# Up product turned round: x stationary, split w_in moving in steps of 512 columns, g transposed behind Mish, and w_out split by TensorE

## The reference

```python
scores = 0.125 * q @ k.T                       # per batch and head, 576 x 576
kth    = 32nd largest score of each row
attn   = softmax(where(scores >= kth, scores, -1e9))
x      = (attn @ v) as 2304 tokens x 512
h      = x @ w_in                              # w_in 512 x 2048
g      = h * tanh(softplus(h))                 # Mish
y      = g @ w_out                             # w_out 2048 x 512
```

## Time and profile before

| | us |
|---|---|
| median of 3 runs | 761.02 (760.97 to 761.91) |
| the profiled execution | 761.13 |
| its span (first to last instruction) | 759.3 |
| busy PE / PEld / DVE / ACT / POOL | 720.5 / 625.3 / 700.5 / 570.3 / 494.3 |

### The profile page before, as it was taken

The page is one execution under the profiler, slowest core; times in us unless marked ns, Lnnn a source line. Parts: engine busy times, 40 slices in busy tenths (PEclk is TensorE's granted clock), DMA queues, the critical chain, the costliest instruction groups (busy, mean ns, idle before and its releaser), DMA issues.

```text
span 759.3 us, 16003 instructions
## 1 busy us (share of the span) xinstructions
PE 720.5 (95%) x6056; PEld 625.3 (82%) x6056; DVE 700.5 (92%) x1512; ACT 570.3 (75%) x942; POOL 494.3 (65%) x590
## 2 busy tenths in 40 slices
PE   4258999999999999999999999999999999999998
PEld 2147888888989898979898989898888888888987
DVE  5999999999999999999999999999999999999600
ACT  3576978787879787878787777878796969687831
POOL 1877858576766666666667585848585858585813
PEclk9998999999999999999999999999999999999999
DMA  7560000031230000111110000001122000000000
GB/s 273 179 214 14 8 22 8 22 104 57 66 102 9 12 20 8 40 33 38 47 52 8 23 8 22 9 22 43 57 78 91 6 22 8 22 2 15 1 15 15
DMA packets 22684, 34.06 MB, mean 45 GB/s; under 512 B 2384, under 2 KB 11600, under 8 KB 22096
## 3 DMA queue, kind: packets, MB, share of 16 engines
q1 hardware_dynamic: 22608, 33.04, 13.3%
HBM read 28.31 MB, written 4.72 MB: 43 GB/s over the span
## 4 chain that ended last, share of the span: by engine, by line
PE 92%; DVE 6%; DMA 0%; issue 0%; ACT 0%; POOL 0%; SPq 0%
PE ps_u L397 35%; PE ps_y L412 27%; PE ps_o L379 10%; PE ps_s L351 9%; PE ps_s L332 9%; DVE left L601 3%; DVE top L607 2%; PE ps_o L372 1%; PE ps_s L328 1%; DVE top L592 1%; DMA q_sb<-q_in 0%; POOL p_sb L674 0%; ACT x_sb L459 0%; ACT xT L499 0%; ACT y_sb L528 0%
## 5 line engine op out<-in xcount | busy, mean ns | idle before, releaser
L607 DVE MAX8 top<-left 128x8 f32<-128x576 f32 x432 | 304.8, 747 | 0.0
L397 PEld LDWEIGHTS ps_u<-xT,win 128*128 128x128 f32 x2304 | 262.5, 192 | 13.8 <-issue 11.1
L397 PE MATMUL ps_u<-xT,win 128*128 128x128 f32 x2304 | 271.8, 277 | 0.7 <-ACT xT L499 0.7
L601 DVE MATCH_REPLACE8 left<-top,left 128x576 f32<-128x576 f32 x288 | 211.8, 743 | 0.0
L659 POOL TENSOR_TENSOR p_sb<-x_sb,p_sb 128x576 f32<-128x576 f32 x144 | 202.4, 1422 | 8.5 <-ACT p_sb L469 8.4
L489 ACT ACTIVATE pT<-ps_s 128x512 f32<-128x512 f32 (+1 forms) x144 | 85.6, 646 | 71.1 <-PE ps_s L351 71.1
L478 ACT ACTIVATE p_sb<-p_sb,neg_max 128x576 f32<-128x576 f32 x144 | 110.6, 769 | 27.7 <-POOL p_sb L659 27.2
L674 POOL TENSOR_SCALAR p_sb<-p_sb,recip 128x576 f32<-128x576 f32 x144 | 106.2, 747 | 35.6 <-DVE recip L582 35.6
L412 PE MATMUL ps_y<-w_hi,g_hi 128*128 128x512 f32 x288 | 117.9, 409 | 0.0
L469 ACT ACTIVATE p_sb<-x_sb,limit 128x576 f32<-128x576 f32 x144 | 105.5, 772 | 12.6 <-POOL limit L649 12.5
L412 PE MATMUL ps_y<-w_hi,g_lo 128*128 128x512 f32 x288 | 112.5, 391 | 0.0
(11 more groups left out here) (30 smaller groups left out, 603.5 us busy)
## 6 DMA issues: line engine op xcount, KB each, us to landing
v_sb<-v_in SPq DMA_DIRECT2D x32, 320.0 KB, 3.5
k_sb<-k_in SPq DMA_DIRECT2D x16, 288.0 KB, 3.3
q_sb<-q_in SPq DMA_DIRECT2D x68, 64.0 KB, 1.8
g_raw<-w_out SPq DMA_DIRECT2D x8, 512.0 KB, 4.4
win<-w_in SPq DMA_DIRECT2D x4, 1024.0 KB, 8.9
y_out<-y_sb SPq DMA_DIRECT2D x16, 256.0 KB, 2.0
y_out<-y_sb SPq DMA_DIRECT2D x4, 128.0 KB, 2.3
q_sb<-q_in SPq DMA_DIRECT2D x1, 256.0 KB, 3.4
```

The source lines that it names most:

```text
L397: mm = pe.matmul(ps_u[:, n % 2, i, :], win[:, k, P * f:P * f + P], xT[:, k, :], start=(k == 0), stop=(k == KC - 1), skip_group_check=True)
L601: dve.match_replace(out=left[:, t, :], in_to_replace=best[:, t, EIGHT * r:EIGHT * r + EIGHT], in_values=x[t] if r == 0 else left[:, t, :], ...
L607: dve.max(best[:, t, EIGHT * r + EIGHT:EIGHT * r + 2 * EIGHT], left[:, t, :]).then_inc(found, 1)
```

## The change

- Up product: `xT` is split into `xT_hi` and `xT_lo` (fp32r, POOL) and is now the weights; w_in is split into `win_hi` and `win_lo`, and moves in steps of 512 columns. One `up(m, j)` is 12 fp32r matmuls of 512 columns and yields token-major sums.
- Mish reads 1024 columns from PSUM and writes `g_tok`; `turn(m, j)` on PE transposes four tiles each (16 a block) back into `ps_u`; `copy_g(m, j)` on ACT copies 512 columns into `raw`, and `split_g(m, j)` on POOL splits them. `g_hi` and `g_lo` hold two of the four groups at a time.
- w_in is split in 8 chunks of 1024 columns (ACT high part, POOL low part). w_out is split in 16 chunks of 512 columns: ACT copies the high part, PE forms w - w_hi in PSUM (`low_w`: a float32 matmul with the identity and an fp32r matmul with its negative), ACT copies it out (`copy_low`), and ACT also issues the loads of chunks 3 to 15. SP's queue starts with k 0, q (three tiles), w_out 0 to 2, w_in 0 and 1, and then k 1 to 3.
- `down(m, 2)` and `down(m, 3)` move into the next round, `down` waits separately for the high and the low part of g.
- XS 4 to 3, QS 4 to 3, `k_sb` 8 to 4 tiles; `left` becomes the duo's `p_sb` slot, so that DVE waits in `topk(s)` for `transposes(s - 3)`; the reciprocals of a block move to 31, 29, 35 and 33 DVE instructions behind the start of their own duo (14 a duo), from 30 each.
- The lists of all engines are in a new order.

```diff
-KS, QS = 2, 4
-XS, PS_, TS, LISTS = 4, 3, 4, 2
-LAG_NORM = 2
+KS, QS = 4, 3
+XS, PS_, TS, LISTS = 3, 3, 4, 2
+INVERSE_AT = (31, 29, 35, 33)
+PER = 14
...
             def up(m, j):
...
-                for i in range(FPG):
-                    f = FPG * j + i
-                    for k in range(KC):
-                        mm = pe.matmul(ps_u[:, n % 2, i, :], win[:, k, P * f:P * f + P], xT[:, k, :],
+                for k in range(KC):
+                    for w in (win_hi, win_lo):
+                        pe.matmul(sums(j), xT_hi[:, k, :], w[:, k, NG * j:NG * j + NG],
...
+                if j == 0:
+                    pe.wait_ge(xTlo_ready, m + 1)
+                for k in range(KC):
+                    mm = pe.matmul(sums(j), xT_lo[:, k, :], win_hi[:, k, NG * j:NG * j + NG],
...
+            def low_w(c):
+                pe.wait_ge(whi_ready, c + 1)
+                if c >= 2:
+                    pe.wait_ge(wlo_ready, c - 1)
+                pe.matmul(w_bank(c), ident[:, :], w_stage(c), start=True, stop=False, skip_group_check=True)
+                pe.matmul(w_bank(c), minus_ident(), w_hi[:, c, :], start=False, stop=True,
...
+            def turn(m, j):
+                pe.wait_ge(mish_ready, 2 * m + j // 2 + 1)
+                for i in range(FPG):
+                    c = NG * (j % 2) + P * i
+                    mm = pe.transpose(ps_u[:, j % 2, i, :], g_tok[:, c:c + P], ident[:, :])
...
+                low_w(12 * m + 18)
+                transposes(4 * m + 3)
+                low_w(12 * m + 19)
                 values(4 * m + 2)
                 values(4 * m + 3)
                 scores(4 * m + 7)
+                down(m - 1, 2)
+                transposes(4 * m + 4)
                 up(m, 0)
-                transposes(4 * m + 4)
+                scores(4 * m + 8)
+                low_w(12 * m + 20)
+                low_w(12 * m + 21)
                 up(m, 1)
-                scores(4 * m + 8)
+                transposes(4 * m + 5)
+                down(m - 1, 3)
+                turn(m, 0)
+                low_w(12 * m + 22)
+                turn(m, 1)
+                scores(4 * m + 9)
+                low_w(12 * m + 23)
+                values(4 * m + 4)
+                low_w(12 * m + 24)
+                values(4 * m + 5)
                 up(m, 2)
-                transposes(4 * m + 5)
                 up(m, 3)
-                scores(4 * m + 9)
-                values(4 * m + 4)
-                values(4 * m + 5)
+                transposes(4 * m + 6)
+                low_w(12 * m + 25)
                 down(m, 0)
-                transposes(4 * m + 6)
+                scores(4 * m + 10)
+                turn(m, 2)
+                turn(m, 3)
+                low_w(12 * m + 26)
+                low_w(12 * m + 27)
                 down(m, 1)
-                scores(4 * m + 10)
-                down(m, 2)
-                down(m, 3)
-                transposes(4 * m + 7)
+                low_w(12 * m + 28)
+                low_w(12 * m + 29)
...
+            def copy_low(c):
+                act.wait_ge(wlow_made, c + 1)
+                if c + WP < FT:
+                    load_w(act, c + WP)
+                act.activation(w_lo[:, c, :], w_bank(c), ACT.Copy).then_inc(wlo_ready, 1)
...
+                left = p_sb[:, s % PS_, :, :]
...
+                        if r == 0 and t == 0 and s >= PS_:
+                            dve.wait_ge(pT_ready, 2 * (s - PS_) + 2)
```

More of the change, by code:

```diff
@@ L104, in in_blocks @@
     return 0 <= m < BLOCKS
-W_SLOTS = (-1, -1, 1, 1, 2, 2, 4, 5)
-def w_chunks_at(s):
-    return [c for c in range(WCHUNKS) if W_SLOTS[c] == s]
+ICHUNKS = 2 * KC
+WP = 3
 def program(nc, k_in, q_in, v, w_in, w_out, y_out):
@@ L448, in splits, with split_in @@
-            def splits(s):
-                for c in w_chunks_at(s):
-                    split_w(c)
+            def split_in(c):
+                if not 0 <= c < ICHUNKS:
+                    return
+                act.wait_ge(in_loaded[c % 2], 16 * (c // 2) + 16)
+                act.activation(in_part(win_hi, c), in_stage(c), ACT.Copy).then_inc(inhi_ready, 1)
+            def split_w(c):
+                if not 0 <= c < FT:
+                    return
+                act.wait_ge(wout_loaded[c % WP], 16 * (c // WP) + 16)
+                act.activation(w_hi[:, c, :], w_stage(c), ACT.Copy).then_inc(whi_ready, 1)
@@ L556, in _ @@
+                penalty(4 * m + 6, 0)
+                split_w(12 * m + 23)
                 mish(m, 0)
+                penalty(4 * m + 6, 1)
                 copy_pT(4 * m + 5, 0)
                 copy_pT(4 * m + 5, 1)
+                copy_low(12 * m + 22)
+                split_w(12 * m + 24)
                 exp(4 * m + 6, 0)
-                copy_up(m, 2)
                 exp(4 * m + 6, 1)
-                copy_up(m, 3)
+                copy_g(m, 0)
+                copy_g(m, 1)
+                copy_y(m - 1)
@@ L576, in _ @@
+                copy_low(12 * m + 28)
+                copy_g(m, 2)
+                split_in(8 * m + 18)
+                copy_low(12 * m + 29)
+                copy_pT(4 * m + 7, 0)
+                copy_pT(4 * m + 7, 1)
+                split_w(12 * m + 30)
+                split_w(12 * m + 31)
         @block.vector
@@ L680, in _ @@
                                pattern=[[-1, P]], channel_multiplier=1).then_inc(ident_ready, 1)
-            for m in range(FIRST_ROUND, BLOCKS):
-                splits(4 * m + 4)
+            for m in range(FIRST_ROUND, BLOCKS + 1):
                 guard(4 * m + 4)
```

341 lines of the change are left out of this document (205 added, 136 removed).

## The result

The changed kernel takes 767.25 us (766.19 to 768.47, 4 runs) beside 761.45 (760.97 to 761.91, 4 runs) for the kernel before on the same chip: ratio 1.0076, 95% interval 1.0063 to 1.0089. It is slower by 5.8 us, inside the range of 757.7 to 768.5, and 5.55 us above the predicted 761.7. The profiled execution took 767.29, its span is 765.4.

The account below looks back on a forecast made before the run. PE at 39.35 us a block bounds before, DVE at 38.8 after. DVE's pace -7.8, longer tail +4.7 and start stalls +3.8 make +0.7 on 761.0: 761.7 us, range 757.7 to 768.5.

Parts of the forecast that it names:

- What bounds before, and what would after: Run of blocks: PE paces at 39.35 us a block before; DVE at 38.8 after, with PE's work at 38.1.
- Up and turn: PE, each block: 14.7 us of float32 up matmuls replaced by 11.4 of fp32r matmuls plus up to 2.0 of transposes.
- The rival at 0.275 for a transpose: PE in blocks: transposes at 0.275 instead of 0.11 us add 2.6 a block, time about 785; chance 0.04.
- The loop in a block: Waits between engines in a block: 0 us of stalls taken, bounds 0 and 0.5 a block, 8 in all.
- The walk: Engine lists stepped through with profiled durations; at the start it gave guard(2) at 53.2 to 56.0, total stall 1.9 to 4.7 us.
- the stage stalls: Rival: in blocks, late exponentials make DVE wait at a reciprocal, 0.2 to 0.5 us a block; 763.5 to 770; chance 0.18.
- The end: After the last duos: longer tail gives back 4.7 us; some 47 us from last MAX8 to end of PE.
- The start: First rounds: weight preparation stalls DVE at the reciprocals of duos 0 to 2; 3.8 us taken, range 0 to 8.
- the start costs more: Rival: first-round stall of 4.8 to 8 us, ACT waiting for w_in that SP releases late; 762.7 to 766; chance 0.17.
- ACT over 90% busy there: First 60 us: ACT busy over 90% where DVE waits 2 to 5 us at the reciprocals of duos 0 to 2.
- the forecast's own bracket: Whole kernel: start stall of 1.6 to 4.7 us and no stall in blocks, 759.5 to 762.5; chance 0.33.
- the start keeps pace: Rival: ACT hides load issues and PE is early at full rate; start stall under 1.6 us; 757.9 to 759.5; chance 0.28.

Follow-up runs that it names:

- the keys first: Changed kernel with SP issuing the loads of k 1 to 3 ahead of the w_out and w_in loads: 764.12 us, ratio 1.0028.
- the two versions with the better queue: Changed kernel, k 1 to 3 before weights, w_in 4 to 7 before q of duos 6 and 7: 760.4 us; also copying duo 5's scores sooner: 760.36 us.
- the second order: Changed kernel, first-round lists reordered: all keys first, scores(2) behind two products, later w_out low-part copies from the sixth on: 761.65 us, ratio 1.0001.
- the first order: Changed kernel, first-round lists reordered: k 1 before weights, w_in before q 6 and 7, scores(2) before products, low-part copies close behind: 771.35 us, ratio 1.0124.
- The first-round kernels: Changed kernel with SP, PE, ACT and POOL lists of rounds -2 and -1 rewritten in three orders: 771.35, 761.65 and 763.53 us.

## Why the prediction was right or wrong

- **What bounds before, and what would after**: right. PE at 39.35 a block gives way to DVE at 38.82 (forecast 38.8). PE's work is 37.8 by the doubled turns (forecast 38.1). PE's spare time doesn't show as waits for GpSimd's p, as the prediction had it: from 325 to 366 us its one recorded wait is 0.45 us, for a copy by ScalarE (346.21).
- **Up and turn**: right. Up groups take 2.72 (1.81 + 0.91) to 2.96 (2.04 + 0.92) in the chain, forecast 2.84 to 2.95; a turn of four transposes is 0.44 (0.88 for eight), forecast 0.44 to 0.5. The rival at 0.275 for a transpose (the Trainium skill, "TensorE: Matmul & The Clock Gate", Part 4: PE-mode transpose) did not come: doubled, 16 took 1.75 and not 4.4 us.
- **The loop in a block**: right. No wait of DVE between 86 us and the last MAX8. The margins are 3.1 us at the reciprocal of a block's third duo, 0.9 at the fourth, 0.4 at the first and 0.5 at the second (in order of time, guards end at 329.65, 340.17, 349.02 and 357.20, reciprocals start at 332.76, 341.08, 349.39 and 357.72). The walk had 0.7 and 0.8 for the second and fourth and named none for the first, which is the smallest. The rival "the stage stalls" did not come, though it was nearer than the walk said.
- **The end**: right in size. From the last MAX8 to the end of PE 46.2 us (716.2 to 762.4), forecast 47.1. The wait for `copy_g` is 0.7 us (744.14 to 744.81, where the next up starts) instead of 0.2; the groups are a little shorter.
- **The start**: this term was mis-sized, 3.8 instead of 9.55, and that is the whole miss: 5.75 us here, 0.4 back from the form, against the 5.55 between 761.7 and 767.25. The rival "the start costs more" named the sign for it, a guard(2) later than 56; it stood at 58.45. Its mechanism, ScalarE waiting for late loads of w_in, is there (2.05 us at 38.38, 0.94 at 48.80), but its own window of 4.8 to 8, up to 766 us, was too short too. With the keys first, guard(2) stands at 55.30 and the waits at duos 0 to 2 are 4.55 us, both inside the walk's own bounds (53.2 to 56.0, 1.9 to 4.7). So of the 5.75, 3.0 are the keys, 2.0 are waits behind duo 2, where the walk ended, and 0.75 lie within its bounds. Four places of the working:
  - The key load behind the weights, taken at 0 because "transfers overlap", cost 3.0. This is the step that failed most. The walk began from a scores(1) done at 11.5; it was done at 14.56. The load was weighed against DVE's need of x(1) at 17.4. What was missed is that scores(1) stands in PE's queue ahead of the first products, so that ACT's list behind copy_x(1) slips with it.
  - The queue of SP: the walk knew that it holds w_in loads behind q loads, and gave this no price of its own. It is another 3.1 of waits (6.52 to 3.39 when lifted).
  - TensorE's products at half rate: charged for the two ahead of scores(2) alone. But after its waits of 4.89 us (42.13) and 4.21 us (55.99) PE is slow again (below), and ScalarE's copies wait: 1.65 at 47.27 and 2.78 at 61.13. Without the low path of w_out 5.7 us of waits go; how much of that is the slow rate isn't shown.
  - The walk ended at duo 2. The "largest stall counts" was sound: 5.20, 1.51 and 0.91 add up to 7.6, and guard(2), at 58.45, is 7.1 us behind its place at 51.3. But 1.93 us came behind it, at duos 3 to 5. Among them is a wait of DVE for p's transposes (0.31 at 66.47), one of the things by which the prediction was to be wrong; it comes once, in the start, and never in the blocks.
- **"ACT over 90% busy there"**: wrong. ScalarE is busy 30.9 of the 40 us from 20 to 60. It waits, for loads (2.99 us in two) and for TensorE (3.4 in four); its own sum of work, on which the start term stood, was not the limit over this stretch. Up to the exponentials of duo 0 it is nearer to it: busy 15.2 of the 18.0 us from 14.6 to 32.6, a length inside the 15.5 to 19.7 that the walk had for it. This is why reordering a queue could give back what an account of ScalarE's time could not see.
- **The side**: slower had the largest chance (0.39), the forecast's own bracket was "same" (0.33). That 767.25 lies inside the stated range is luck: the range reaches above 766 only for the stalls of the stage, and these did not come. The time of the rival on the other side ("the start keeps pace", 757.9 to 759.5) is reached only by the kernel without preparation (757.72); the two versions with the better queue stay at 760.4, some 3 us above that kernel.

## What to carry to other kernels

When a change moves preparation into the start, walk each in-order queue with its waits and not each engine's sum: here the engines had time to spare, and the order of SP's loads alone made 1.0076 or 0.9989 of the same work. Look first for a small load that the first products need behind bulk loads (3.0 us here), and for a bulk load behind one that waits for a later step (3.1 us here). Check a supposed cause by an identity over all variants, such as span less the bounding engine's waits; where it holds, the loss lies in these waits and nowhere else, and single edits must then show what causes them.

## What the runs showed of the hardware

- PE at half rate after waits of 4.89 and 4.21 us. In the changed kernel the granted clock by stretches (columns: window, length, then busy time and instructions of PE, PEld, DVE, ACT and POOL, granted clock, DMA share, GB/s):

```profile
37.00:42.00 5.00, 0.23 (x3) 0.00 (x0) 5.00 (x10) 3.62 (x6) 4.01 (x3) 0.56 0.33 133
42.00:44.40 2.40, 2.27 (x9) 1.32 (x9) 0.89 (x3) 2.01 (x5) 0.74 (x2) 0.50 0.00 0
44.40:48.00 3.60, 3.60 (x7) 1.79 (x6) 3.60 (x9) 1.79 (x3) 3.43 (x5) 0.52 0.60 185
48.00:50.00 2.00, 1.62 (x11) 0.97 (x9) 2.00 (x5) 1.20 (x2) 0.36 (x2) 1.00 0.88 299
```

After 4.89 us without work (up to 42.13) the clock is 0.50, the lower level of 1.2 GHz, for the scores (2.29 instead of 1.24) and the products behind them, and 1.00 (2.4 GHz) again from 48 on. The scores after the wait of 4.21 us, at 55.99, also take 2.29. So here a late step made the next ones slow. Shorter waits are no clear sign: after 2.76 us (36.06) nine transposes took 1.17, after 2.73 us in the second order (40.50) they took 2.15.

- The granted clock in the records doesn't always show the slow rate: from 12.0 to 14.5 the column says 1.00 while the scores take 2.29 (12.27). In the kernel without the low part of w_out, where TensorE is busy 16.4 of the 40 us from 20 to 60, it says 1.00 for all of them, and the scores at 27.51, 38.67 and 52.19 take 2.29 each. There the duration of a known group is the measure.
- A load took longer at the start, among others. A key tile of 288 KB took 8.2 us behind the weights, 3.1 in the median of all; a w_out chunk of 256 KB took 5.4 at 18.25 in the first order, beside a median of 3.2 for the chunks that ScalarE loads into the same tile there.
- The first-round kernels with all the preparation scatter more (759.1 to 763.9 for the second order) than the kernel before (761.0 to 762.3, run beside it). That loads of the first microseconds land differently is only a guess; no run shows it.
